# The products of the b weights' rests in a fused mixing and two-MLP kernel, run as two 64-row matmuls

## The reference

```
w   = softmax(weight_gen, last axis)
mix[b, s, h, g] = sum over k of w[b, s, h, k] * x[b, s + k - 6, h, g]   (zeros ahead of the sequence)
h1  = mix @ moe_w_in;    g1 = max(0.01 * h1, h1);          y1  = g1 @ moe_w_out
h2  = y1 @ moe2_w_in;    g2 = where(h2 > 0, h2, exp(h2)-1); out = g2 @ moe2_w_out
```

## Time and profile before

| | |
|---|---|
| Times of three runs | 1210.0, 1211.51, 1213.1 us (median 1211.51) |
| Profiled execution: span | 1212.5 us; first work at 0.7 us, last at 1210.2 us |
| TensorE matmul (PE) busy | 1186.3 us, 98% |
| Weight loads (PEld) busy | 973.8 us, 80% |
| VectorE (DVE) busy | 814.6 us, 67% |
| ScalarE (ACT) busy | 745.8 us, 62% |
| GpSimd (POOL) busy | 354.3 us, 29% |
| Chain that ended last | PE 91%, DVE 5%, DMA 2%, ACT 1% |

### The profile page before, as it was taken

How to read it: one execution, slowest core, us unless ns; L and a number is a source line. 1 busy time by engine, 2 the same in 40 slices (tenths; PEclk the granted TensorE clock), 3 DMA queues, 4 the chain that set the end, 5 groups by cost and what they waited for, 6 DMA issues and landing times.

```text
span 1212.5 us, 14538 instructions
## 1 busy us (share of the span) xinstructions
PE 1186.3 (98%) x5208; PEld 973.8 (80%) x5208; DVE 814.6 (67%) x778; ACT 745.8 (62%) x815; POOL 354.3 (29%) x216
## 2 busy tenths in 40 slices
PE   6798999999999999999999999999999999999998
PEld 4586888888888888888888888888888888888887
DVE  6877675666757666675766757666675766756555
ACT  3465757656575665747656575665747656575675
POOL 4725051150703307051150703307051150700000
PEclk8999999999999999999999999999999999999999
DMA  8221102011120101102010120211002010110001
GB/s 193 75 84 37 26 27 76 27 49 26 39 62 26 62 30 58 26 26 75 26 49 26 39 62 26 62 33 55 26 32 70 26 49 26 39 26 26 14 16 37
DMA packets 42723, 54.24 MB, mean 45 GB/s; under 512 B 3733, under 2 KB 32531, under 8 KB 42193
## 3 DMA queue, kind: packets, MB, share of 16 engines
q1 hardware_dynamic: 42704, 54.00, 15.0%
HBM read 36.29 MB, written 17.69 MB: 45 GB/s over the span
## 4 chain that ended last, share of the span: by engine, by line
PE 91%; DVE 5%; DMA 2%; ACT 1%; SPq 0%; issue 0%; POOL 0%; ACTq 0%; POOLq 0%
PE hidden L495 46%; PE y_b L524 9%; PE y_b L525 9%; PE y_a L531 9%; PE y_a L529 9%; PE y_a L530 9%; DMA raw_d<-in_moe_w_out_dram 2%; DVE hid_lo L933 1%; DVE hidden L894 1%; ACT hid_hi L792 1%; DVE up_b_lo L814 1%; DVE up_a_lo L814 1%; DVE dn L342 0%; DVE dn L341 0%; DVE in_b L860 0%; DVE in_a_lo L858 0%
## 5 line engine op out<-in xcount | busy, mean ns | idle before, releaser
L933 DVE TENSOR_TENSOR hid_lo<-hidden,hid_hi 128x1024 fp32r<-128x1024 f32 x254 | 311.0, 1224 | 241.7 <-ACT hid_hi L792 241.7
L792 ACT ACTIVATE hid_hi<-hidden 128x1024 fp32r<-128x1024 f32 x254 | 260.8, 1027 | 328.8 <-DVE hidden L894 202.1
L897 DVE SCALAR_TENSOR_TENSOR hidden<-act,hidden 128x1024 f32<-128x1024 f32 x129 | 157.5, 1221 | 100.2 <-ACT act L767 98.1
L281 POOL TENSOR_TENSOR mix<-xw,wk 128x768 f32<-128x768 f32 x15 | 23.3, 1551 | 685.8 <-DVE wk L840 683.3
L495 PE MATMUL hidden<-in_a_hi,up_a_hi 128*128 128x512 f32 x510 | 201.3, 395 | 12.4 <-DVE hid_lo L933 11.5
L524 PE MATMUL y_b<-hid_hi,dn 128*128 128x512 f32 x512 | 199.5, 390 | 1.3 <-DVE dn L342 1.3
L525 PE MATMUL y_b<-hid_lo,dn 128*128 128x512 f32 x512 | 199.4, 389 | 0.0
L495 PE MATMUL hidden<-in_a_hi,up_a_lo 128*128 128x512 f32 x510 | 199.3, 391 | 0.0
L495 PE MATMUL hidden<-in_a_lo,up_a_hi 128*128 128x512 f32 x510 | 199.2, 391 | 0.0
L529 PE MATMUL y_a<-hid_hi,dn 128*128 128x512 f32 x512 | 199.2, 389 | 0.0
L531 PE MATMUL y_a<-hid_lo,dn 128*128 128x512 f32 x512 | 199.2, 389 | 0.0
(11 more groups left out here) (100 smaller groups left out, 1139.6 us busy)
## 6 DMA issues: line engine op xcount, KB each, us to landing
xw<-in_x_dram SPq DMA_DIRECT2D x14, 960.0 KB
raw_b<-squares_out SPq DMA_DIRECT2D x60, 96.0 KB, 2.2
out_dram<-staged SPq DMA_DIRECT2D x15, 384.0 KB, 2.3
squares_in<-prod SPq DMA_DIRECT2D x56, 96.0 KB, 2.0
squares_out<-ya SPq DMA_DIRECT2D x15, 256.0 KB, 2.0
raw_a<-squares_in SPq DMA_DIRECT2D x14, 256.0 KB, 2.8
raw_d<-in_moe_w_out_dram SPq DMA_DIRECT2D x2, 1536.0 KB, 14.1
raw_a<-in_moe_w_in_dram SPq DMA_DIRECT2D x2, 1024.0 KB, 9.1
```

Of the source, the lines that this page charges most:

```text
L281: ops.tensor_tensor(dst, src, w, ALU.mult).then_inc(done, 1)
L792: nc.scalar.activation(hid_hi[:, s % 2, :], hidden[:, s % 2, :], ACT.Copy).then_inc(s_hi, 1)
L897: nc.vector.scalar_tensor_tensor(out=h, in0=a, scalar=-1.0, in1=h, op0=ALU.add, op1=ALU.max).then_inc(done, 1)
L933: nc.vector.tensor_tensor(hid_lo[:, s % 2, :], h, hid_hi[:, s % 2, :].bitcast(f32), ALU.subtract).then_inc(s_lo, 1)
```

## The change

`up_b_lo` holds, in half as many columns, the rests for tile 0 of each step on partitions 0 to 63 and those for tile 1 on partitions 64 to 127. A second copy of the rounded b input stands on partitions 64 to 127 of a new tile `in_b_up`; ACT writes it just before it writes `in_b`. Each tile keeps four full matmuls. The fifth, `up_b_lo`·`in_b`, becomes a 64-row matmul; the two of a step stand together at the end of `up` and use different rows of the array and different banks of PSUM (`up_pair`). The tiny lo·lo term is no longer formed. DVE makes the rests of a quarter with two subtractions on 64 partitions and 256 columns each.

```
-        up_b_lo = [sb(f"up_b_lo{m}", [P, F], f32r) for m in (0, 1)]
+        up_b_lo = [sb(f"up_b_lo{m}", [P, F // 2], f32r) for m in (0, 1)]
+        in_b_up = [sb(f"in_b_up{n}", [P, T], f32r) for n in (0, 1)]
 def up(m, src, g, s):
     for i in (0, 1):
         cols = slice((2 * s + i) * P, (2 * s + i + 1) * P)
-        dst = hidden[:, s % 2, i * T:(i + 1) * T]
-        pairs = ((up_a_hi, in_a_hi), (up_a_lo, in_a_hi), (up_b_hi, in_b), (up_b_lo, in_b), (up_a_hi, in_a_lo))
+        pairs = ((up_a_hi, in_a_hi), (up_a_lo, in_a_hi), (up_b_hi, in_b), (up_a_hi, in_a_lo))
         for n, (w, v) in enumerate(pairs):
-            last = nc.tensor.matmul(dst, w[m][:, cols], v[src][:, :], start=(n == 0), stop=(n == len(pairs) - 1))
-        if halved(g) and i == 0:
-            last.then_inc(s_up1, 1)
-    last.then_inc(s_up, 1)
+            nc.tensor.matmul(hidden[:, s % 2, HALF[i]], w[m][:, cols], v[src][:, :], start=(n == 0), stop=False)
+    half = up_pair(m, src, s)
+    if halved(g):
+        half[0].then_inc(s_up1, 1)
+    half[1].then_inc(s_up, 1)
+
+def up_pair(m, src, s):
+    cols = slice(s * P, (s + 1) * P)
+    return [
+        nc.tensor.matmul(hidden[:, s % 2, HALF[0]], up_b_lo[m][0:D2, cols], in_b[src][0:D2, :], start=False, stop=True),
+        nc.tensor.matmul(hidden[:, s % 2, HALF[1]], up_b_lo[m][D2:P, cols], in_b_up[src][D2:P, :], start=False, stop=True),
+    ]
 def up_first():
     ...
     product(0, up_b_hi, in_b, start=False, stop=False)
-    product(0, up_b_lo, in_b, start=False, stop=True).then_inc(s_up1, 1)
     product(1, up_a_hi, in_a_lo, start=False, stop=False)
     product(1, up_b_hi, in_b, start=False, stop=False)
-    product(1, up_b_lo, in_b, start=False, stop=True).then_inc(s_up, 1)
+    half = up_pair(0, input_of(0, 0), 0)
+    half[0].then_inc(s_up1, 1)
+    half[1].then_inc(s_up, 1)
 # mlp1_input_hi (and mlp2_input_hi with yb[0] and input_of(1, c))
+    nc.scalar.activation(in_b_up[n][D2:P, :], b, ACT.Copy)
     nc.scalar.activation(in_b[n][0:D2, :], b, ACT.Copy).then_inc(s_xhi, 1)
 # split_up, the b part of quarter q
+    for i in (0, 1):
+        rows = slice(i * D2, (i + 1) * D2)
+        def tiles(ap):
+            return ap[rows, cols].rearrange("p (t i n) -> p t i n", i=2, n=P)[:, :, i, :]
+        lo = up_b_lo[m][rows, q * F // QUARTERS // 2:(q + 1) * F // QUARTERS // 2].rearrange("p (t n) -> p t n", n=P)
+        last = nc.vector.tensor_tensor(lo, tiles(raw_b), tiles(up_b_hi[m]).bitcast(f32), ALU.subtract)
+    last.then_inc(s_uplo, 1)
```

More of the change, by code:

```diff
@@ L694, in mlp2_input_hi @@
                 else:
+                    nc.scalar.activation(in_b_up[input_of(1, c)][D2:P, :], yb[0][:, :], ACT.Copy)
                     nc.scalar.activation(in_b[input_of(1, c)][0:D2, :], yb[0][:, :], ACT.Copy).then_inc(s_mhi, 1)
@@ L810, in split_up @@
                 for n in parts:
-                    lo, hi, raw = ((up_a_lo, up_a_hi, raw_a), (up_b_lo, up_b_hi, raw_b))[n]
                     dve.wait_ge(s_uphi, 2 * (QUARTERS * m + q) + 1 + n)
-                    nc.vector.tensor_tensor(lo[m][:, cols], raw[:, cols], hi[m][:, cols].bitcast(f32), ALU.subtract).then_inc(s_uplo, 1)
+                    if n == 0:
+                        nc.vector.tensor_tensor(up_a_lo[m][:, cols], raw_a[:, cols], up_a_hi[m][:, cols].bitcast(f32),
+                                                ALU.subtract).then_inc(s_uplo, 1)
+                        continue
+                    for i in (0, 1):
[5 more added lines that the diff above has]
+                    last.then_inc(s_uplo, 1)
             def mixing_share():
```

## The result

The changed kernel takes 1264.72 us (median of 4 runs, 1264.24 to 1266.1) against 1212.3 us before (4 runs): ratio 1.0429, 95% interval 1.0412 to 1.0446. The forecast was 1276 us, +65; it became +52. Its profiled execution has a span of 1264.3 us, 51.8 more than the one before.

A forecast was written before the change was run, and what follows sets the result against it. TensorE's summed starts were taken as the bound after about 111 us. Per step -0.227 + 0.38 + 0.11 = +0.26 us, +62 over 240 steps, plus 1 and 2, gave 1276 us; range 1192 to 1310.

The forecast's parts named there:

- What bounds: DVE sets the pace up to about 111 us; after that the sum of TensorE's starts alone decides the end.
- The slot saved: In each step's `up`, two 64-row matmuls side by side take one slot instead of two: -0.227 us per step.
- Two changes of shape: Going from 128-row to 64-row matmuls and back costs 0.19 us each, 0.38 a step; ends 0.24 and 0.55.
- The second load of the pair: Both 64-row weight loads in the open, one behind the other: lower half's matmul 0.11 us later; ends 0 and 0.227.
- R1: Rival, faster: shape changes free and the pair side by side; about 1176 us (1150 to 1200), chance 0.16.
- The copies and the split: Added ACT copy mostly hidden, +1 us; DVE's halved weight subtractions and the first 16 steps, +2 us.
- R3: Rival, much slower: the pair's matmuls run one after the other, +0.38 us a step, about 1306 us; chance 0.08.
- R4: Rival: gaps of 0.3 us a step could lower TensorE's granted clock; given nothing of its own.
- The signs: Expected in the changed profile: delayed 64-row load, steps of 4.79 us, TensorE windows not full, longer DVE and ACT waits.

The follow-up runs named there:

- e3: Changed kernel with both 64-row matmuls of a step on rows 0 to 63, in all steps but first and last: 1320.24 us.
- e4: Changed kernel with each 64-row matmul right behind its own tile's four full ones, so four shape changes a step and no pair: 1427.03 us.
- e2: Changed kernel with only the upper of the two 64-row matmuls in all steps but the first and last: 1258.01 us.
- e1: Changed kernel with the two 64-row matmuls run as two 128-row ones in all steps but the first and last: 1217.84 us.
- e6: Changed kernel with one full 128-row matmul in place of the pair in all steps but the first and last: 1169.73 us.
- e7: Changed kernel with two pairs back to back in even steps and none in odd ones (the last step keeps its pair): 1218.94 us.
- e8: Changed kernel with the rounded b weights' products also as 64-row pairs, three pairs in one excursion: 1266.98 us.
- b1: Kernel before the change, its last eight transpositions sorted to have two row-shape changes instead of seven: 1212.54 us against 1213.74.
- e9: Changed kernel without the two ACT copies into `in_b_up`; the lower 64-row matmul reads the lower half of `in_b`: 1264.0 us.

## Why the prediction was right, and where it missed

- **What bounds:** right. From step 18 on the end moved by the sum of TensorE's starts: 0.196 us in 238 steps.
- **The slot saved,** -0.227: right. e3 puts both halves on one set of rows and loses 0.22.
- **Two changes of shape,** +0.38: measured 0.40 at the pair (1.08 us for three slots), and 0.40 for each of the two excursions of e4. Their making was right too: the load 0.31 us after the start before it (0.32 forecast), and a weight load paid in the open. Carrying the 0.09 us gap over from 64- and 128-column transpositions and adding this stream's own load worked; the bare sum of rows 5 and 6, 0.24, would have missed by 40%. There is luck in it all the same. The 0.06 us that I read as an open load is the amount by which the record of L588 is longer than that of L589, but both load in the open, and L588 streams 64 columns more, 0.11 against 0.05 us, which explains the 0.06 as well. So rows 5 didn't give the gap of 0.09 by itself. The stream does now: 0.31 us less the 0.21 that 512 columns take at 2.4 GHz is 0.10.
- **The second load of the pair,** +0.11: this is the step that failed, "both loads are in the open, one behind the other". The two loads start 0.01 us apart, and e2 puts the whole second half at 0.03 us, hardly any of it at the pair. I took the interval of two loads into the same rows, and e3, where the rows are the same, does show 0.11. With 0.01 to 0.03 in its place the step comes to +0.16 to +0.18 and the time to 1254 to 1258 us. That is 7 to 11 us under the measured 1264.7, so the forecast was as near as it was partly because this term, some 20 us too high, was met by others too low: 0.40 for 0.38 is 5 us in 240 steps, and the copies and the split are 2 us more. The section of the Trainium skill cited for R1 (TensorE: Matmul & The Clock Gate, Part 3: starts some 4 ns apart) was the better source for this term: the trace agrees, with 0.01 us or less.
- **The copies and the split,** +3 in all: +5.3 (e1). The split is 4.0 of it, within the 0.5 to 5 stated; the copies' 0.7 to 2.1 us can't be told from nothing, which agrees with a hidden copy but doesn't prove it.
- **R1's worth** was understated, 36 us for 48 (e6), by a floor read from a duration instead of from start to start. Half of R1's condition came true, the pair running side by side; the changes of shape weren't free, so none of its gain arrived. **R3** needed the same rows (e3). **R4:** the clock stayed at 1.00 in the stream.
- **The signs:** the load 0.31 us behind the start before it, `up` of step 16 ahead of 116 us (115.62) and ACT's longer wait for TensorE came true. Not so TensorE's windows: they are full, 77.00 of 77.00 us, since a record covers the wait for its weights. The first load of `down` comes 0.42 us after the second 64-row matmul, not some 0.3; the sum's own terms, 0.11 of load, 0.21 of streaming and the gap of 0.09, give 0.41. A step lasts 4.74 us, not 4.79.

## What to carry to other kernels

Every change between 128 and 64 rows in this stream of matmuls cost about a slot (0.20 us with 512 columns at full clock): the next load doesn't run ahead across it, and the matmul waits for its load. Two 64-row matmuls on different rows do run as one. So a single pair between full matmuls saves one slot and pays two changes; two pairs an excursion break even (e7). With three or more it should gain a slot for each further pair by these prices, since e8's pairs follow each other every 0.23 us, but no run compares that with as many full matmuls. Where shapes already alternate, sorting them helps (0.7 us in b1's trace). Look for it not in the busy share but in the distance from a matmul's start to the next weight load.

## What the runs showed of the hardware that was not expected

- Two weight loads into different rows start together (621.26 and 621.27), while two into the same rows are 0.11 us apart (e3).
- Behind an excursion the next nine full matmuls start slightly wider apart, 2.06 us after one pair and 2.07 to 2.08 after two, against 2.04. With a single 64-row matmul a step there is no such tail (e2, 2.040 us in the mean), while two into the same rows have it (e3, 2.064) and two that stand apart have more, behind the second (e4, 2.10). So it comes with the second 64-row matmul of a step and not with the two running together. No run shows why.
- DVE's subtraction on 64 partitions and 256 columns takes 0.41 us alone and up to 2.05 beside GpSimd (e9).
